# Local attention and two feed-forward layers in fp32: token tiles of 512 and a first one of 256, attention for two blocks at a time in parts of the array

## The chip, the cores and the metric

One core of a Trainium2 chip runs the whole kernel. The metric is the device time of one execution in microseconds (us). A profiled execution gives the rows quoted below; all times in a row are us unless it says ns.

## The reference

Three stages over 2304 tokens (4 sequences of 576) of 512 features (8 heads of 64):

```python
# 1. causal attention with a window of 64 keys
scores = q @ k.T / sqrt(64); mask = (rel >= 0) & (rel < 64)      # rel = query position - key position
x = softmax(where(mask, scores, -1e9)) @ v                       # heads side by side: (2304, 512)
# 2. first feed-forward layer
h = maximum(x @ w_in1, 0); x = (h * h) @ w_out1                  # 512 -> 2048 -> 512
# 3. second feed-forward layer
h = x @ w_in2; out = (h * cos(h)) @ w_out2                       # 512 -> 2048 -> 512
```

Everything is fp32. The feed-forward products are made of three passes each: both operands are split into a high part (rounded by a cast to fp32r) and a low part (the rest), and high*high, high*low and low*high are added in PSUM.

## The kernel before

**Work and tiles.** The tokens are in 6 tiles of 384 (TILE), a tile in 6 attention blocks of 64 queries (QT). The hidden 2048 features are in 16 chunks of 128 (CH). All four split weights of one layer stay in SBUF; the second layer's replace the first's during the last tile of the first. Features are in partitions, tokens in columns.

**Attention of a block** of 64 queries looks at 128 keys (the block's own and the 64 before). `qk` (L333) multiplies, for each of 4 head pairs, a stationary matrix of 128x128 in which the queries of one head fill the upper left quarter and those of the other the lower right, with zeros elsewhere, by 128 key columns. `mask_max` (L669, L674) on DVE scales, masks and takes the row maximum, `exps` (L496) on ACT exponentiates and sums, `invert` and `norm` (L680, L682, L703) on DVE divide, `turn` (L346) on PE transposes, `copy_turned` (L504) on ACT copies to SBUF, `pv` (L361) on PE multiplies the values of both heads (128 keys x 128) by 128 columns of weights, of which the two diagonal 64x64 quarters are used, and `x_high` (L513, ACT) and `x_low` (L689, DVE) split those into x_hi and x_lo, each in two pieces of 64 partitions.

**Feed-forward.** `up` (L371) is 12 matmuls of 384 columns for one chunk; `down1` (L401) is 12 matmuls of 384 columns with the weights stationary; `down2` (L427) is 9 matmuls of 512 columns with the activations stationary, so its output has tokens in partitions. Between them stand, in layer 1, `relu1` (L536, ACT), `square` (L724, DVE), `g_high` (L542, ACT) and `g_low` (L729, DVE); in layer 2 `count_turns` (L563, ACT), three DVE operations (L762, L765, L768), `cosines` (L571, ACT), `times_cos` (L774, DVE), `g_high` and `g_low`.

**What sets the order.** Each engine's program is written out by hand, and semaphores join them. PE does the attention of all 6 blocks of tile 0 first, and only then `up1(0, 0)`. From there a step is `up1(f)`, `down1(f - 2)`, and in tiles 0 to 4 one of `turn` and `qk`, or `pv`, for the next tile's blocks in between. In tile 0 each step also has two weight pieces of 256 KB to take in: SP loads them through three buffers (L248), ACT casts the high part (`w_high`, L529), DVE subtracts (`w_low`, L709). The tiles 1 to 4 of layer 1 and 0 to 4 of layer 2 are hardware loops. Layer 1's result goes to DRAM in fp32 (`store_x2`) and is loaded and split again for layer 2.

```python
for i in range(QT + 4):                       # PE, tile 0
    ...
    if 4 <= i:
        pv(0, i - 4, v0_bank[(i - 4) % 4])
up1(0, 0, 0)
up1(0, 1, 0)
tile1(0, 0, 1)
```

Of the kernel before, what the change touches and what calls it, by code (L numbers as in the profile page):

```python
# [6 lines left out]
def attention_ffn_ffn(nc, q_blocks, k_cols, v_rows, w_in1, w_out1, w_in2, w_out2, x2_dram, out):  # L25
# [5 lines left out]
    P = 128  # L31
    NBLK, _, PAIRS, BLK = q_blocks.shape
    TOKENS, D = v_rows.shape
    WIN = 2 * BLK
    HD = P // 2
    SEQ_BLOCKS = 9
    SCALE = float(HD) ** -0.5
    MASKED = -1000000000.0
    CH = w_in1.shape[0]
    KC = D // P  # L40
    TILE = 384
    TILES = TOKENS // TILE
    QT = TILE // BLK
    TB = TILE // P
    LAG = 2
    L2 = TILES * CH
    SLOTS = 3
    WSLOTS = 3
# [5 lines left out]

    ANGLE_MAX, ANGLE_MIN = HALF_PI - 1e-6, -3 * HALF_PI + 1e-6

    with ExitStack() as ctx:
# [9 lines left out]

        w_in_hi = sb("w_in_hi", [P, KC, CH * P], f32r)
        w_in_lo = sb("w_in_lo", [P, KC, CH * P], f32r)
        w_out_hi = sb("w_out_hi", [P, CH, D], f32r)  # L70
        w_out_lo = sb("w_out_lo", [P, CH, D], f32r)
        w_raw = sb("w_raw", [P, WSLOTS, D])

        x_hi = sb("x_hi", [P, 2, KC, TILE], f32r)
        x_lo = sb("x_lo", [P, 2, KC, TILE], f32r)

        g_hi = sb("g_hi", [P, 2, TILE], f32r)
        g_lo = sb("g_lo", [P, 2, TILE], f32r)

        SLOT = 3 * D  # L80
        work = sb("work", [P, 2 * SLOT])
        relu = work[:, 0:2 * TILE].rearrange("p (s c) -> p s c", s=2)
        act = work[:, 2 * TILE:4 * TILE].rearrange("p (s c) -> p s c", s=2)
        y_stage = work[:, 4 * TILE:8 * TILE]

        arena = sb("arena", [P, SLOTS * (SLOT + PAIRS * WIN) + 2 * PAIRS * P])
        at = [0]

        def carve(n, start=None):
            if start is not None:  # L90
                at[0] = start
            at[0] += n
            return arena[:, at[0] - n:at[0]]

        def qkv(place):

            q, k = (place[:, n * D:(n + 1) * D].rearrange("p (a c) -> p a c", a=PAIRS) for n in range(2))
            return q, k, place[:, 2 * D:3 * D]

        slots = [qkv(carve(SLOT)) for _ in range(SLOTS)] + [qkv(work[:, n * SLOT:(n + 1) * SLOT]) for n in range(2)]  # L100

        slot0 = [0, 1, 2, 3, 4, 0]
        TILE0_USED = [6, 2, 3]
        prob = carve(SLOTS * PAIRS * WIN).rearrange("p (s a c) -> p s a c", s=SLOTS, a=PAIRS)
        prob_t = carve(2 * PAIRS * P).rearrange("p (s a c) -> p s a c", s=2, a=PAIRS)
        x2_raw = carve(KC * TILE, 0).rearrange("p (k c) -> p k c", k=KC)
        turns = carve(2 * TILE).rearrange("p (s c) -> p s c", s=2).bitcast(i32)
        cosine = carve(2 * TILE).rearrange("p (s c) -> p s c", s=2)
# [3 lines left out]
        neg_max = sb("neg_max", [P, SLOTS, PAIRS])  # L112
        row_sum = sb("row_sum", [P, SLOTS, PAIRS])
        inv_sum = sb("inv_sum", [P, SLOTS, PAIRS])
# [5 lines left out]
        y_bank = [ps(f"y{d}") for d in range(KC)]  # L120
        s_bank = ps("scores")
        t_bank = ps("turned")
        h2_bank = h_bank + [s_bank, t_bank]

        s0_bank, t0_bank, v0_bank = (s_bank, y_bank[0]), (t_bank, y_bank[1]), y_bank[2:] + h_bank
# [4 lines left out]
        zeros_set = sem("zeros_set")  # L130
# [14 lines left out]
        pv_done = sem("pv_done")  # L145
        xhi_set = sem("xhi_set")
        xlo_set = sem("xlo_set")
        w_loaded = [sem(f"w_loaded{n}") for n in range(WSLOTS)]
        whi_set = sem("whi_set")
        wlo_set = sem("wlo_set")  # L150
        up_done = sem("up_done")
# [789 lines left out]
```

## Time and profile before

| | |
|---|---|
| Time, median of 3 runs (lowest to highest) | 911.57 us (910.73 to 912.2) |
| The profiled execution: its own time, its span | 912.68 us, 910.9 us |
| PE (matmul) busy | 890.9 us, 98% |
| PEld (weight load) busy | 847.9 us, 93% |
| DVE busy | 524.8 us, 58% |
| ACT busy | 394.2 us, 43% |
| DMA | 54.68 MB, mean 60 GB/s |
| First feed-forward matmul begins | 30.97 us |

A timeline row is: start, duration, engine, source line, operation, output and inputs, partitions x columns, count; in square brackets the idle time before it and what ended it. The duration of a matmul holds the time through the array, in which the next ones already run: what a matmul costs in a dense stretch is the distance from its start to the next start. One fp32 matmul of the program is two instructions in the trace (x8 for four), an fp32r matmul or a transpose is one.

### The profile page before, as it was taken

The page shows a single profiled execution, that of the slowest core. Times are in us where ns is not written, and L with a number is a line of the kernel's source. Part 1 is how long each engine was busy: PE and PEld are TensorE (multiplying, and loading weights), DVE is VectorE, ACT ScalarE, POOL GpSimd, SP SyncE. Part 2 cuts the span into 40 slices and gives each one's busy share as a digit, 9 for nine tenths or more (in the row PEclk, how much of TensorE's full clock was granted, in tenths as well). Part 3 has the DMA queues.
Part 4 walks back from the last instruction along what each step waited for, and adds up shares of the span by engine and source line. Part 5 has one row for each costly group of instructions (what it writes and reads, how often), then busy time and mean ns, then how long its engine had stood idle before and what let it go on. Part 6 is the DMA issues. An engine that isn't in the chain of part 4 may idle for free.

```text
span 910.9 us, 14676 instructions
## 1 busy us (share of the span) xinstructions
PE 890.9 (98%) x5040; PEld 847.9 (93%) x5040; DVE 524.8 (58%) x1028; ACT 394.2 (43%) x967; POOL 2.4 (0%) x13
## 2 busy tenths in 40 slices
PE   6899899999999999999999999999999999999998
PEld 6798899999999999999999999999899999989997
DVE  7666644535444443544375766665665666666664
ACT  6665534434433443344255533433433433433433
POOL 1000000000000000000000000000000000000000
PEclk9999999999999999999999999999999999999999
DMA  6544412221221121120354310010000010000000
GB/s 196 157 121 146 150 59 59 58 59 63 58 60 60 58 58 58 63 58 0 105 158 124 124 35 1 35 35 0 35 35 0 35 35 0 35 0 0 36 1 35
DMA packets 57119, 54.68 MB, mean 60 GB/s; under 512 B 22592, under 2 KB 40512, under 8 KB 57088
## 3 DMA queue, kind: packets, MB, share of 16 engines
q1 hardware_dynamic: 56560, 54.15, 19.1%
q8 instruction: 18, 0.29, 0.1%
q10 hardware_dynamic: 528, 0.13, 0.1%
q14 instruction: 13, 0.11, 0.0%
HBM read 44.83 MB, written 9.44 MB: 60 GB/s over the span
## 4 chain that ended last, share of the span: by engine, by line
PE 90%; DVE 3%; DMA 3%; ACT 2%; issue 1%; SPq 1%
PE h L371 31%; PE y L427 22%; PE y L401 19%; PE turned L371 6%; PE scores L371 6%; PE turned L361 3%; PE scores L333 2%; PE turned L346 1%; DMA w_raw<-w_in 1%; ACT arena L496 1%; DMA w_raw<-w_out 1%; DMA arena<-q_blocks 0%; DVE arena L669 0%; DVE neg_max L674 0%; DVE g_lo L729 0%
## 5 line engine op out<-in xcount | busy, mean ns | idle before, releaser
L371 PE MATMUL h<-x_hi,w_in_hi 128*128 (+1 forms) x576 | 199.2, 346 | 1.7 <-DVE x_lo L689 1.7
L371 PE MATMUL h<-x_hi,w_in_lo 128*128 (+1 forms) x576 | 193.9, 337 | 0.0
L371 PE MATMUL h<-x_lo,w_in_hi 128*128 (+1 forms) x576 | 193.6, 336 | 0.0
L729 DVE TENSOR_TENSOR g_lo<-work,g_hi 128x384 fp32r<-128x384 f32 x192 | 106.4, 554 | 135.2 <-ACT g_hi L542 135.2
L542 ACT CAST g_hi<-work 128x384 fp32r<-128x384 f32 x192 | 97.2, 506 | 104.6 <-PE y L401 84.1
L401 PE MATMUL y<-g_hi,w_out_lo 128*128 128x384 f32 x384 | 128.4, 334 | 0.0
L401 PE MATMUL y<-g_lo,w_out_hi 128*128 128x384 f32 x384 | 128.3, 334 | 0.0
L401 PE MATMUL y<-g_hi,w_out_hi 128*128 128x384 f32 x384 | 128.3, 334 | 0.0
L427 PE MATMUL y<-w_out_hi,g_lo 128*128 128x512 f32 x288 | 113.9, 396 | 0.0
L427 PE MATMUL y<-w_out_lo,g_hi 128*128 128x512 f32 x288 | 113.7, 395 | 0.0
L371 PEld LDWEIGHTS h<-x_hi,w_in_hi 128*128 128x128 f32 x576 | 109.0, 189 | 4.0 <-DVE x_lo L689 1.9
L427 PE MATMUL y<-w_out_hi,g_hi 128*128 128x512 f32 x288 | 111.9, 389 | 0.0
L371 PEld LDWEIGHTS h<-x_lo,w_in_hi 128*128 128x128 f32 x576 | 108.8, 189 | 2.0
L371 PEld LDWEIGHTS h<-x_hi,w_in_lo 128*128 128x128 f32 x576 | 108.5, 188 | 0.0
L571 ACT ACTIVATE arena<-work,half_pi 128x384 f32<-128x384 f32 x96 | 59.3, 617 | 109.0 <-DVE work L768 109.0
L536 ACT ACTIVATE work<-h 128x384 f32<-128x384 f32 x96 | 47.2, 491 | 134.7 <-PE h L371 134.6
L724 DVE TENSOR_TENSOR work<-work 128x384 f32<-128x384 f32 x96 | 53.4, 556 | 65.8 <-ACT work L536 65.6
L401 PEld LDWEIGHTS y<-g_hi,w_out_hi 128*128 128x128 f32 x384 | 72.1, 188 | 0.0
L401 PEld LDWEIGHTS y<-g_hi,w_out_lo 128*128 128x128 f32 x384 | 72.1, 188 | 0.0
L401 PEld LDWEIGHTS y<-g_lo,w_out_hi 128*128 128x128 f32 x384 | 72.1, 188 | 0.0
L427 PEld LDWEIGHTS y<-w_out_hi,g_lo 128*128 128x128 f32 x288 | 54.0, 187 | 11.5
L427 PEld LDWEIGHTS y<-w_out_lo,g_hi 128*128 128x128 f32 x288 | 54.0, 187 | 9.2
(96 smaller groups left out, 1179.7 us busy)
## 6 DMA issues: line engine op xcount, KB each, us to landing
arena<-k_cols SPq DMA_DIRECT2D x33, 256.0 KB, 3.4
arena<-v_rows SPq DMA_DIRECT2D x33, 256.0 KB, 3.4
w_raw<-w_in SPq DMA_DIRECT2D x32, 256.0 KB, 3.6
w_raw<-w_out SPq DMA_DIRECT2D x32, 256.0 KB, 2.7
x_tiles<-work SPq DMA_DIRECT2D x6, 768.0 KB, 3.3
arena<-x_tiles SPq DMA_DIRECT2D x6, 768.0 KB, 4.4
arena<-q_blocks SPq DMA_DIRECT2D x68, 64.0 KB, 2.3
out<-work SPq DMA_DIRECT2D x5, 768.0 KB, 3.5
```

The source lines that it names most:

```text
L333: mm = pe.matmul(bank[:, a * WIN:(a + 1) * WIN], q[:, a, :], k[:, a, :], start=True, stop=True)
L346: mm = pe.transpose(bank[:, a * P:(a + 1) * P], prob[:, i % SLOTS, a, :], ident[:, :])
L361: mm = pe.matmul(bank[:, a * P:(a + 1) * P], v[:, a * P:(a + 1) * P], prob_t[:, i % 2, a, :], start=True, stop=True)
L371: mm = pe.matmul(bank[:, 0:TILE], w[:, k, cols], x_at(x, par, k), start=(n == 0), stop=(n == 3 * KC - 1))
L401: mm = pe.matmul(y_bank[d][:, 0:TILE], w[:, f, cols], g[:, f % 2, :], start=(f == 0 and n == 0), stop=(f == CH - 1 and n == 2))
L427: mm = pe.matmul(y_bank[b][:, 0:D], g[:, f % 2, cols], w[:, f, :], start=(f == 0 and n == 0), stop=(f == CH - 1 and n == 2))
L496: e = nc.scalar.activation(p, p, ACT.Exp, bias=neg_max[:, i % SLOTS, a:a + 1], accum_out=row_sum[:, i % SLOTS, a:a + 1])
L536: nc.scalar.activation(relu[:, f % 2, :], h_bank[f % 2][:, 0:TILE], ACT.Relu).then_inc(relu_set, 1)
L542: nc.scalar.copy(g_hi[:, f % 2, :], act[:, f % 2, :]).then_inc(ghi_set, 1)
L571: nc.scalar.activation(cosine[:, f % 2, :], relu[:, f % 2, :], ACT.Sin, bias=half_pi[:, 0:1]).then_inc(cos_set, 1)
L724: nc.vector.tensor_tensor(act[:, f % 2, :], relu[:, f % 2, :], relu[:, f % 2, :], ALU.mult)\
L729: nc.vector.tensor_tensor(g_lo[:, f % 2, :], act[:, f % 2, :], g_hi[:, f % 2, :].bitcast(fp32), ALU.subtract).then_inc(glo_set, 1)
```

## The change

The tokens are in one tile of 256 and four of 512. In the 256 tile two chunks are handled in one step, side by side in one PSUM bank, so that ACT and DVE work on 512 columns everywhere. Attention is done for two blocks at a time (a duo). `qk` multiplies 64x64 stationary matrices by 128 columns, the one head in the upper left and the other in the lower right quarter of the array, with no zero filling. `pv` multiplies 128x64 stationary matrices by 64 columns, the heads in the two column halves. One `x_high` and one `x_low` on all 128 partitions serve a duo. PE does only duos 0 and 1 (the 256 tile) and `qk(2)` before the first `up1`; duos 2 to 5 come in the 8 steps of the 256 tile, four duos in the 16 steps of each 512 tile after that.

Weights come in pieces of 512 KB through two buffers, 16 for a layer; the first three are split by POOL (`w_split`). A duo's queries and keys are one DMA of 640 KB, its values one of 512 KB. ACT squares (`g_high1`) from the relu result itself, and DVE squares in place for `g_low`. Layer 1's result is split into x_hi and x_lo right from PSUM (`y_high`, `y_low`); its last two tiles stay in SBUF and are the first of layer 2, the others go through DRAM already split. All loops are written out. The range of each engine's program: PE 3901 rows (1964 before), ACT 494 (413), DVE 746 (539), SP 84 (204).

```diff
-    TILE = 384
-    LAG = 2
-    SLOTS = 3
-    WSLOTS = 3
+    WIDE = 512
+    HALF = 256
+    FIRST_DUOS = 2
+    RAW1, RAW2 = 2, 4
+    SIZE = [HALF] + [WIDE] * ((TOKENS - HALF) // WIDE)
+    ORDER = [TILES - 2, TILES - 1] + list(range(1, TILES - 2)) + [0]
...
-                for a in range(PAIRS):
-                    mm = pe.matmul(bank[:, a * WIN:(a + 1) * WIN], q[:, a, :], k[:, a, :], start=True, stop=True)
+                for a in range(PAIRS):
+                    for b in range(2):
+                        for head in range(2):
+                            rows, to = slice(head * HD, (head + 1) * HD), head
+                            mm = pe.matmul(score_bank(2 * d + b)[to * HD:(to + 1) * HD, a * WIN:(a + 1) * WIN],
+                                           q_at[d % 2][rows, a, b * BLK:(b + 1) * BLK],
+                                           k_at[d % 2][rows, a, b * BLK:b * BLK + WIN],
+                                           start=True, stop=True, tile_position=(head * HD, to * HD))
...
-                for a in range(PAIRS):
-                    mm = pe.matmul(bank[:, a * P:(a + 1) * P], v[:, a * P:(a + 1) * P],
-                                   prob_t[:, i % 2, a, :], start=True, stop=True)
+                for b in range(2):
+                    pe.wait_ge(prob_t_set, 2 * d + b + 1)
+                    for a in range(PAIRS):
+                        for head in range(2):
+                            place = head
+                            mm = pe.matmul(pv_bank(d)[head * HD:(head + 1) * HD,
+                                                      (b * PAIRS + a) * BLK:(b * PAIRS + a + 1) * BLK],
+                                           v_at[d % 2][:, b, a * P + head * HD:a * P + (head + 1) * HD],
+                                           prob_t[:, b, a, place * BLK:(place + 1) * BLK],
+                                           start=True, stop=True, tile_position=(0, head * HD))
...
+            for s in range(WSTEPS):
+                up1(s)
+                if s % 2 == 0 and s > 0:
+                    pv(FIRST_DUOS + s // 2 - 1)
+                if s % 2 == 0 and s < WSTEPS - 2:
+                    qk(FIRST_DUOS + s // 2 + 1)
+                if s % 2 == 1:
+                    turn(2 * FIRST_DUOS + s - 1)
+                    turn(2 * FIRST_DUOS + s)
+                if s > 0:
+                    down1(s - 1)
...
+            def w_split(n):
+                _, hi, lo, raw = piece(n)
+                pool.wait_ge(w1_loaded[n % RAW1], 16 * (n // RAW1 + 1))
+                nc.gpsimd.tensor_copy(hi, raw).then_inc(whi_first, 1)
+                pool.wait_ge(whi_first, n + 1)
+                nc.gpsimd.tensor_tensor(lo, raw, hi.bitcast(fp32), ALU.subtract).then_inc(wlo_first, 1)
```

How the instructions stand. PE from its first instruction to the first feed-forward matmul, before (L333 is qk, L346 turn, L361 pv, L371 up):

```order
L333 MATMUL scores<-arena 128x128 x4
L333 MATMUL y<-arena 128x128 x4
L333 MATMUL scores<-arena 128x128 x4
L333 MATMUL y<-work 128x128 x4
...
L346 MATMUL y<-ident,arena 128x128 x4
L361 MATMUL y<-arena,work 128x128 x4
L361 MATMUL y<-arena 128x128 x4
L371 MATMUL h<-x_hi,w_in_hi 128x384
```

and the same place in the change (L341 is qk, L355 turn, L365 pv, L385 up):

```order
L341 MATMUL y<-arena 64x128 x32
L355 MATMUL scores<-ident,arena 128x128 x4
L355 MATMUL turned<-ident,arena 128x128 x4
L365 MATMUL y<-arena 64x64 x16
L355 MATMUL scores<-ident,act 128x128 x4
L355 MATMUL turned<-ident,act 128x128 x4
L365 MATMUL y<-arena 64x64 x16
L341 MATMUL y<-arena 64x128 x16
L385 MATMUL h<-x_hi,w_in_hi 128x256
```

Four blocks instead of six stand ahead of the first `up`, and the scores of two more; the qk of one duo is 16 matmuls of 128 columns where two blocks had 8, its pv 16 of 64 columns where two blocks had 8 of 128.

PE in the second tile of layer 1, change: the qk of duo 6 stands between the 12 matmuls of `up` and the 12 of the next chunk's, all of 512 columns now:

```order
L385 MATMUL h<-x_hi,w_in_lo 128x512
L341 MATMUL scores<-arena 64x128 x2
L341 MATMUL turned<-arena 64x128 x2
L341 MATMUL scores<-arena 64x128 x2
L341 MATMUL turned<-arena 64x128 x2
...
L385 MATMUL h<-x_hi,w_in_hi 128x512
```

There each of `qk` and `pv` is entered from and left to full-array matmuls once for a duo.

DVE in an odd step of the change's first tile (L708 is square, L715 g_low, L672 and L677 mask_max, L703 w_low, L682 to L687 norm):

```order
L708 TENSOR_TENSOR act<-act 128x512
L715 TENSOR_TENSOR g_lo<-act,g_hi 128x512
L672 SCALAR_TENSOR_TENSOR arena<-y,masks 128x512
L677 TENSOR_REDUCE neg_max<-arena 128x4
L703 TENSOR_TENSOR w_in_lo<-arena,w_in_hi 128x1024
L703 TENSOR_TENSOR w_out_lo<-arena,w_out_hi 128x1024
L682 TENSOR_SCALAR row_sum<-row_sum 128x4
L684 RECIPROCAL inv_sum<-row_sum 128x4
L687 TENSOR_TENSOR arena<-arena,inv_sum 128x512
```

Before, a block's softmax and two pieces of 512 columns stood in a pair of steps with two squares and two g_lows; now a block's softmax and two pieces of 1024 columns stand in every step.

## Rows read from the trace of the kernel before

**Rows 1.** The page, busy us, share of the span, instructions.

```profile
PE 890.9 (98%) x5040; PEld 847.9 (93%) x5040; DVE 524.8 (58%) x1028; ACT 394.2 (43%) x967; POOL 2.4 (0%) x13
```

**Rows 2.** Windows, PE alone: length, busy (matmuls), granted clock, DMA share, GB/s.

```profile
4.60:13.60 9.00, 8.14 (x33) 1.00 0.85 218
31.00:110.00 79.00, 73.41 (x449) 0.98 0.52 156
110.00:200.00 90.00, 90.00 (x566) 1.00 0.20 61
600.00:700.00 100.00, 100.00 (x503) 1.00 0.07 24
```

**Rows 3.** Waits of PE: total us, times, longest.

```profile
PE scores L333 <- DMA arena<-q_blocks: 4.8, 2, 4.6
PE turned L346 <- DVE x_lo L689: 4.6, 3, 1.7
```

**Rows 4.** Timeline of PE, layer 1 with attention in between.

```profile
123.33 1.05 PE L333 MATMUL scores<-arena 128*128 128x128 f32 x8
124.14 0.42 PE L371 MATMUL h<-x_hi,w_in_hi 128*128 x1
124.39 0.34 PE L371 MATMUL h<-x_lo,w_in_hi 128*128 x1
...
132.55 0.60 PE L346 MATMUL turned<-ident,arena 128*128 128x128 f32 x4
132.98 1.06 PE L333 MATMUL scores<-arena 128*128 128x128 f32 x8
...
138.04 1.05 PE L361 MATMUL turned<-arena 128*128 128x128 f32 x8
138.85 0.42 PE L371 MATMUL h<-x_hi,w_in_hi 128*128 x1
139.11 0.34 PE L371 MATMUL h<-x_lo,w_in_hi 128*128 x1
```

**Rows 5.** Timeline of PE, dense stretches of layer 1 and at layer 2's end.

```profile
126.48 0.33 PE L401 MATMUL y<-g_lo,w_out_hi 128*128 128x384 f32 x1
...
128.56 0.33 PE L371 MATMUL h<-x_lo,w_in_hi 128*128 x1
...
902.26 0.39 PE L427 MATMUL y<-w_out_lo,g_hi 128*128 128x512 f32 x1
...
907.25 0.39 PE L427 MATMUL y<-w_out_hi,g_lo 128*128 128x512 f32 x1
```

**Rows 6.** Timeline of PE, the start, and the first `up`.

```profile
4.58 2.04 PE L333 MATMUL scores<-arena 128*128 128x128 f32 x8 [4.58 <-DMA arena<-q_blocks]
...
30.97 0.69 PE L371 MATMUL h<-x_hi,w_in_hi 128*128 128x384 f32 x1 [1.73 <-DVE x_lo L689]
...
33.38 0.52 PE L371 MATMUL h<-x_lo,w_in_hi 128*128 128x384 f32 x1
33.70 0.48 PE L371 MATMUL h<-x_hi,w_in_lo 128*128 128x384 f32 x1
```

**Rows 7.** Timeline of weight loads after a qk.

```profile
124.11 0.19 PEld L371 LDWEIGHTS h<-x_hi,w_in_hi 128*128 128x128 f32 x1
124.22 0.19 PEld L371 LDWEIGHTS h<-x_lo,w_in_hi 128*128 128x128 f32 x1
```

**Rows 8.** The page, DMA issues: count, KB each, us to landing.

```profile
w_raw<-w_out SPq DMA_DIRECT2D x32, 256.0 KB, 2.7
...
arena<-x_tiles SPq DMA_DIRECT2D x6, 768.0 KB, 4.4
```

**Rows 9.** Timeline of DVE and ACT, tile 0.

```profile
39.25 0.69 DVE L669 SCALAR_TENSOR_TENSOR arena<-scores,masks 128x512 f32<-128x512 f32 x1
40.58 0.55 DVE L724 TENSOR_TENSOR work<-work 128x384 f32<-128x384 f32 x1
...
43.55 0.62 ACT L529 CAST w_out_hi<-w_raw 128x512 fp32r<-128x512 f32 x1
```

More of the change, by code:

```diff
@@ L95, in qkv @@
[L95 to L105, printed above, removed]
@@ new lines, in _ @@
+            qk(0)
+            qk(1)
+            pe.wait_ge(ident_set, 1)
+            turn(0)
+            turn(1)
+            pv(0)
+            turn(2)
+            turn(3)
+            pv(1)
+            qk(2)
+            for s in range(WSTEPS):
+                up1(s)
[8 more added lines that the diff above has]
+                    down1(s - 1)
@@ L869, in _ @@
[L869 to L880 removed]
+            mask_max(0)
@@ new lines, in _ @@
+            mask_max(1)
+            norm(0)
+            mask_max(2)
+            norm(1)
+            mask_max(3)
+            norm(2)
+            x_low(0)
+            norm(3)
+            x_low(1)
+            mask_max(4)
+            mask_max(5)
+            norm(4)
+            for s in range(WSTEPS):
+                d = FIRST_DUOS + s // 2
+                if s == 0:
+                    norm(5)
+                square(s)
+                g_low(s)
+                if s % 2 == 0 and s > 0:
+                    x_low(d - 1)
+                if d + 1 < EARLY_DUOS:
+                    t = 2 * (d + 1) + s % 2
+                    mask_max(t)
+                for n in pieces1_of(s):
+                    w_low(n)
+                if d + 1 < EARLY_DUOS:
+                    norm(2 * (d + 1) + s % 2)
@@ new lines, in _ @@
+            x_low(EARLY_DUOS - 1)
+            for g in range(first1[1], G1):
+                j, s, _ = steps1[g]
+                d = START[min(j + 1, TILES - 1)] // (2 * BLK) + s // 4
+                if j + 1 < TILES:
+                    if s % 4 == 0:
+                        mask_max(2 * d)
+                    if s % 4 == 1:
+                        norm(2 * d)
+                square(g)
+                g_low(g)
+                if s == 0:
+                    y_low(j - 1)
+                if j + 1 < TILES:
+                    if s % 4 == 0:
+                        mask_max(2 * d + 1)
+                    if s % 4 == 1:
+                        norm(2 * d + 1)
+                    if s % 4 == 3:
+                        x_low(d)
+                else:
+                    for n in pieces2_of(s):
+                        w_low(n)
@@ new lines, in _ @@
+            for g in range(G2):
+                i, s, _ = steps2[g]
+                if g > 0:
+                    g_low(G1 + g - 1)
+                angles(g)
+                if g == 0:
+                    y_low(TILES - 1)
+                if g < 2:
+                    for n in pieces2_of(2 * WSTEPS + g):
+                        w_low(n)
+                if s == 1 and i > 0:
+                    y2_copy(i - 1, 1)
+                    y2_copy(i - 1, 3)
+                times_cos(g)
+            g_low(G1 + G2 - 1)
```

1138 lines of the change are left out of this document (522 added, 616 removed).

## The prediction

> **What bounds the kernel now.** The page says it first: PE is busy 890.9 of 910.9 us [rows 1]. The windows say where it isn't: from 110 us on every window is full, between 31 and 110 us (most of tile 0) 5.6 us are lost, and before 31 us PE only does attention [rows 2]. The waits of PE name the gaps: the first loads, then turn waiting for DVE's x_lo [rows 3]. So the end is set by the sum of PE's own work, plus the start until the first `up`. DVE and ACT matter in the start and in tile 0 alone. I therefore price everything by the distance between matmul starts, not by the durations in the rows.
>
> Those distances. In layer 1 twelve matmuls of 384 columns take from 126.48 to 128.56, 0.1733 each; at the end 22 of 512 columns take from 902.26 to 907.25, 0.2268 each [rows 5]. 384 columns at 2.4 GHz are 0.160, 512 are 0.2133: in both cases 0.0133 is left over. So a matmul costs its columns and 13.3 ns, and wider matmuls save the 13.3 ns. A step of layer 2 (21 matmuls) takes 100 x 21 / 503 = 4.175 [rows 2], against 12 x 0.1733 + 9 x 0.2268 = 4.12, so 0.05 of disturbance, which I leave as it is. In layer 1 a step is 24 x 0.1733 = 4.16.
>
> Attention of a block: `qk` begins at 123.33, the second matmul after it at 124.39; less one 0.173 it costs 0.89. `pv` the same way (138.04, 139.11) 0.90. `turn` to the next `qk` (132.55, 132.98) 0.43 [rows 4]. Together 2.21 a block.
>
> The sum closes: 30.97 to the first `up` [rows 6], 30 blocks x 2.21 = 66.3, 96 steps x 4.16 + 96 x 4.175 = 800.2, the first nine matmuls at 0.32 instead of 0.173 (1.3) [rows 6], 5.6 idle [rows 2], is 904.4; the last matmul ends at 907.64 [rows 5], so 3.2 stays unexplained, and 3.3 goes from there to the end of the span. I carry both over.
>
> **The start.** The zero filling by DVE and the many small loads go away, but the first qk needs 640 KB where the old one had three small loads, and the second duo's 640 KB come in beside it. A load of 256 KB takes 2.7, of 768 KB 4.4 [rows 8], so 512 KB more cost 1.7; 1280 KB should take about 6.1 after an issue at 0.7, and qk(0) starts at about 6.7 instead of 4.58. PE is slow there: four matmuls (eight instructions) take 2.04 [rows 6] instead of 0.89, and the first `up` matmuls are 0.32 apart [rows 6], which is 384 columns at 1.2 GHz: the lower clock level by its spacing, though the granted clock of that window reads 1.00 [rows 2]. Four blocks' scores end near 13.7, as before. From there it is a chain through DVE and ACT, of 1.33 for a mask and maximum (39.25 to 40.58 [rows 9]), some 1.6 for four exponentials, 1.0 for a norm. Laid out in the written order, norm(3) ends near 21.7, pv(1) near 24.3, its x_low near 25.7. qk(2) waits for that and costs 1.8: first `up` at 27.5. Before it was 30.97, with six blocks done instead of four.
>
> **Attention after the start**, in 16 duos. Turns: 8 transposes each, 0.86, 13.8 in all. qk: 16 matmuls of 128 columns in a duo. If the two quarters run side by side that is the time of 8, 1.77; 15 of them 26.6. If they don't, twice that. pv: 16 matmuls of 64 columns. With halves side by side and everything in step with the columns 0.89; if weight loads or the halves come one after the other, 1.79, the same as two old pv. Rows show two weight loads of 128 columns 0.11 apart [rows 7], so 64 columns could be loaded in 0.055, four of them to a pair of matmuls: that alone would give 1.76 if the two halves' loads can't overlap. I take 1.3, between the ends: 20.8 in all (14.2 to 28.6).
>
> Entering and leaving these modes is 4 changes a duo, 64 in all. The trace has no such change. Its nearest rows are the change from fp32 to fp32r, after which the first matmul is 0.25 instead of 0.173 from the next, so 0.08 (124.14 to 124.39 [rows 4]), and an emptied array: a matmul of 384 columns lasts 0.33, 0.16 more than its distance [rows 5]. With the weight load of 0.19 [rows 7] not hidden either it would be 0.35. Nothing below: a change can't save time. I take 0.12, between the two nearest: 7.7 (0 to 22). The Trainium skill (TensorEngine Tiling (Array Packing), section Key Properties) says that changing the tiling mode drains TensorE. With a full 0.16 a change the sum would be 2.5 higher. No run yet shows the drain.
>
> **Feed-forward.** The columns stay the same. The matmuls become fewer: 5 x 16 x 12 instead of 6 x 16 x 12 for each layer's `up` and for `down1`, 576 less in all, at 13.3 ns: 7.7 saved, 800.2 becomes 792.5. This needs 256 columns to take 0.120. An fp32 instruction of qk has its own weight load and takes 0.111 (0.89/8 [rows 4]), so the load alone allows it; the other end is that the loads need the 0.173 they have now, which would cost the 576 matmuls of 256 columns 31. I take 0.120. The cold matmuls after the start stay, 1.3.
>
> **First tile, 8 steps.** PE has per step 48 x 0.120 = 5.76 and some 2.2 of attention, 8.0. DVE and ACT now pass a block through in each step: square and g_low 1.35, mask 1.33, exponentials 1.7, w_high 0.95, w_low twice 1.1 each, norm 1.0, and x_low in every second step; these follow one another across both engines (exponentials wait for the mask, w_low for w_high, the norm stands behind both w_low) and add up to about 9.0. The 1024-column costs are estimates, from 512 columns at 0.69 and 384 at 0.55, 0.62 for the cast [rows 9]. For six steps PE loses 1.0 each, with hops 7 in all, where 5.6 were lost before.
>
> **Later tiles.** ACT and DVE have 5.5 a step and need about 3.3 at most; y_high and y_low at a tile's end have the 2.7 of an `up` and a `down`. Nothing. At the very end the chain from the last `up` through cos to g_low is some 0.1 longer per operation, and the change no longer issues the last two `up` together: 0.5.
>
> **The sum:** 27.5 + 13.8 + 26.6 + 20.8 + 7.7 + 792.5 + 1.3 + 7 + 0.5 + 3.2 + 3.3 = 904.2 of span, against 910.9. The profiled execution's own time was 1.8 over its span and 1.1 over the median of the runs, so 904.9 us.
>
> **The rivals.** *A, all overlaps, changes free:* pv at 0.89 and no cost of a change, 904.9 - 6.6 - 7.7 = 890.6. For it: the trace shows weight loads hidden everywhere. Against: such short matmuls stand nowhere in it. 18%.
>
> *B, changes dear:* 0.35 each and pv at 1.79: 904.9 + 14.7 + 7.8 = 927.4, slower. For it: the 13.3 ns that are left at every weight change say that a handover costs something even without a change of mode. Against: attention's fp32 stretches are entered for 0.08. 12%.
>
> *C, the two quarters of qk don't run side by side,* and this is the one on the other side that I can name a place for: qk 3.55 a duo. It costs 26.6 after the start, and in the start, on the path, twice 3.55 (at the lower level) and 1.8: 940.4. Its point: from half an overlap on (13 + 4) the change loses. In this kernel both quarters write the same bank at the same time, in different partitions, which the old qk never did. The Trainium skill (TensorEngine Tiling, Gotcha 1: PSUM Pressure) says that different row tiles can't access one PSUM bank simultaneously, and by that rule it would be this case; the same skill (TensorE: Matmul & The Clock Gate, Part 3) gives 10.6 times for 16 tiles, with (section Why this matters for your kernels) a bank for each row of tiles. Nothing in the trace decides it. 12%.
>
> *D, tile 0 starved:* two buffers of 512 KB; a piece is loaded (3.6, from the loads of 256 and 768 KB [rows 8]) between w_low in one step and w_high in the next, some 7 apart. SP's queue is written in order, and POOL's splits of the first three pieces, for which the trace has no price, stand ahead of pieces 3 and 4. If each of six steps lacks 2 more: 904.9 + 12 = 916.9. For it: waits of this sort exist [rows 3]. Against: 218 GB/s were reached [rows 2], about 170 are needed. 8%.
>
> The forecast keeps 50%.
>
> **How the numbers follow.** A measurement of this kernel can tell about 0.2% from no change, 1.8 us: faster means below 909.7. The forecast's own range is 897 to 912 (pv and changes towards their ends, 2 to 12 lost in tile 0), of which some 8 parts in 10 are faster. With A that gives 0.61 faster; some of D's mass and the forecast's upper edge give 0.07 the same; B, C, most of D and the rest 0.32 slower. The range for 8 in 10 takes A and B in and leaves C out: 889 to 928.
>
> **What would show it.** In the profile after: the first `up` at 27 to 28; distances of 0.120 and 0.2268 in the feed-forward stretches; a qk of a duo at 1.8 from start to next `up`, a pv at 0.9 to 1.8; PE idle of 3 to 10 in the first tile and nearly none behind it. Wrong it would be if qk takes 3.5 (C), if the matmul next to a change starts more than 0.2 late (B), if 256 columns take over 0.13, or if the windows of the first 100 us show more than 15 idle (D).

## The result and the profile after

The change makes the kernel slower by 0.4%: 915.67 us, the median of 8 runs (913.68 to 918.51), beside 911.74 (910.48 to 913.07, 8 runs) of the kernel before. The ratio is 1.0044, with a 95% interval of 1.0029 to 1.006. The profiled execution took 915.88 us, its span is 913.7 us. The forecast was 904.9 and faster: the time lies in its range of 889 to 928, the direction is wrong.

The page first, the line that answers to [rows 1]:

```profile
PE 877.4 (96%) x5040; PEld 736.4 (81%) x5040; DVE 474.4 (52%) x761; ACT 363.1 (40%) x762; POOL 12.7 (1%) x19
```

PE is busy 13.5 less than before, and yet the span is 2.8 longer. So the work did become cheaper, and more than that went into waiting: PE is idle for 36.3 of its span, where it was for 20.0. The windows say where. PE alone, columns as in [rows 2], first of the kernel after:

```profile
0.00:30.00 30.00, 12.59 (x144) 0.84 0.58 211
30.00:60.00 30.00, 25.03 (x246) 0.87 0.35 114
60.00:90.00 30.00, 23.17 (x220) 0.94 0.37 124
90.00:120.00 30.00, 26.80 (x256) 0.94 0.43 150
118.00:510.80 392.80, 392.25 (x2365) 1.00 0.20 66
510.80:910.50 399.70, 399.51 (x1850) 1.00 0.07 24
```

and the same of the kernel before:

```profile
30.00:60.00 30.00, 27.88 (x166) 0.94 0.57 175
60.00:90.00 30.00, 28.14 (x179) 1.00 0.43 126
90.00:120.00 30.00, 27.42 (x168) 1.00 0.45 134
```

From 118 us on PE is full, as forecast. From 30 to 120 it is idle for 15.0 where it was idle for 6.6, its granted clock is 0.87 to 0.94, and the DMA engines move *less* than before (114 and 124 GB/s in the first two windows, 175 and 126 before). Something upstream of both is late. The waits of PE in the whole span, against [rows 3]:

```profile
PE y L341 <- DMA arena<-qk_duos: 13.6, 3, 6.2
PE h L385 <- DVE w_in_lo L703: 6.5, 3, 2.2
PE scores L355 <- DVE arena L687: 4.4, 1, 4.4
PE turned L355 <- DVE arena L687: 3.6, 1, 3.6
...
PE scores L355 <- DVE x_lo L697: 1.0, 1, 1.0
```

One of the three waits for queries and keys is the start (6.2). The other two (7.4) and the three for w_in_lo (6.5) are in the first tile, and [rows 3] had neither there.

**Two marks in PE's timeline** cut the sum into pieces, the first `up` and the first `up` of tile 1:

```profile
30.07 3.68 PE L341 MATMUL y<-arena 64*64 64x128 f32 x32 [1.50 <-DVE x_lo L697]
33.68 0.58 PE L385 MATMUL h<-x_hi,w_in_hi 128*128 128x256 f32 x1
...
115.12 0.40 PE L385 MATMUL h<-x_hi,w_in_hi 128*128 128x512 f32 x1
```

By the forecast's terms they stand at 27.5 and 97.5 (27.5, 8 steps x 5.76, 1.3 and 7, and 15.6 of attention: 3 qk, 4 pv, 4 duos' turns and their 14 mode changes). Measured they are at 33.68 and 115.12. So the start lost 6.2 and the first tile 11.4. From the second mark to the end of the span the terms give 806.7, and it took 798.6: 8.1 better than forecast. 904.2 + 6.2 + 11.4 - 8.1 = 913.7.

**The start.** POOL splits the first pieces (CAST, then TENSOR_TENSOR); here are its rows

```profile
9.93 2.35 POOL L829 TENSOR_TENSOR w_in_lo<-arena,w_in_hi 128x1024 fp32r<-128x1024 f32 x1
...
13.34 2.34 POOL L829 TENSOR_TENSOR w_in_lo<-arena,w_in_hi 128x1024 fp32r<-128x1024 f32 x1
...
17.21 2.35 POOL L829 TENSOR_TENSOR w_out_lo<-arena,w_out_hi 128x1024 fp32r<-128x1024 f32 x1
```

and those of DVE beside them:

```profile
10.04 0.69 DVE L672 SCALAR_TENSOR_TENSOR arena<-y,masks 128x512 f32<-128x512 f32 x1 [9.12 <-PE y L341]
...
13.44 0.18 DVE L684 RECIPROCAL inv_sum<-row_sum 128x4 f32<-128x4 f32 x1
13.65 2.58 DVE L687 TENSOR_TENSOR arena<-arena,inv_sum 128x512 f32<-128x512 f32 x1
...
17.47 2.11 DVE L682 TENSOR_SCALAR row_sum<-row_sum 128x4 f32<-128x4 f32 x1
```

The norm (L687) took 2.58 where it takes 0.69 elsewhere, and a TENSOR_SCALAR of 4 columns 2.11 where it takes 0.17. Both begin while a subtraction of POOL runs. The small one ends with it (19.58 and 19.56), the norm 0.55 after it (16.23 and 15.68), as if it had begun only then. The mask (10.04), in the middle of the first subtraction, keeps its 0.69, and so does the reciprocal (13.44, inside the second) its 0.18. Together the norm and the small operation lost 3.8 in DVE's queue; how much of that reached the first `up` runs 1 and 10 show. The other large piece is `qk(2)`, at 30.07: 3.6 instead of 1.8, at the lower clock level (granted clock 0.50 from 30.1 to 33.6).

**The first tile.** One step of it. PE's rows first:

```profile
64.56 0.60 PE L355 MATMUL turned<-ident,arena 128*128 128x128 f32 x4
...
70.19 0.39 PE L385 MATMUL h<-x_hi,w_in_hi 128*128 128x256 f32 x1 [2.16 <-DVE w_in_lo L703]
...
79.07 3.41 PE L341 MATMUL y<-arena 64*64 64x128 f32 x32 [4.67 <-DMA arena<-qk_duos]
```

then DVE's

```profile
64.84 0.69 DVE L672 SCALAR_TENSOR_TENSOR arena<-y,masks 128x512 f32<-128x512 f32 x1 [4.21 <-PE scores L355]
...
68.91 1.23 DVE L703 TENSOR_TENSOR w_in_lo<-arena,w_in_hi 128x1024 fp32r<-128x1024 f32 x1 [2.66 <-ACT w_in_hi L544]
```

ACT's

```profile
66.29 0.40 ACT L512 ACTIVATE arena<-arena,neg_max 128x128 f32<-128x128 f32 x1 [8.42 <-DVE neg_max L677]
...
67.85 1.03 ACT L544 CAST w_in_hi<-arena 128x1024 fp32r<-128x1024 f32 x1
```

and SP's queue:

```profile
70.16 0.33 SPq L252 DMA_DIRECT2D arena<-w_in  x1
...
71.67 1.21 SPq L243 DMA_DIRECT2D arena<-v_duos  x1
72.92 0.43 SPq L238 DMA_DIRECT2D arena<-qk_duos  x1
```

Read in order of time this is a circle. The next duo's mask (64.84) waits for this duo's `turn`, because `prob` (the tile that holds the masked scores and then the weights of the softmax) has room for one duo: DVE stands idle for 4.21 before it and ACT for 8.42. `w_high` is written behind the exponentials, and waits there, though its piece lies in SBUF. `w_low` (68.91) waits for `w_high`, and PE's next `up` for `w_low` (2.16). Only `w_low`'s end frees the piece's buffer, so SP issues the next piece's load then (70.16, 71.30), and the loads of v and of the next queries and keys, which wait for nothing of that, stand behind it in the queue: they go out at 71.67 and 72.92, and `qk` waits 4.67 for them. That qk makes the next turn late, and the turn the next mask. From one turn to the one two steps on (64.56 to 88.71) it takes 24.2, where the forecast's terms give some 18. Behind some of the waits PE runs at the lower clock level: the `qk` at 79.07 takes 3.41 instead of 1.96, and after the wait of 2.16 before 47.93 fifteen matmuls of 256 columns start 0.213 apart, which is 256 columns at 1.2 GHz (granted clock 0.50 from 48.0 to 51.3). Not behind all of them: after the wait of 2.16 before 70.19 they start 0.12 apart at once (granted clock 1.00 from 70.2 to 73.0). What decides between the two, these rows don't show.

**The steady tiles** went by the terms. PE around a pv and a qk, layer 1:

```profile
213.45 0.39 PE L385 MATMUL h<-x_hi,w_in_lo 128*128 128x512 f32 x1
213.77 1.15 PE L365 MATMUL scores<-arena 128*64 128x64 f32 x32
214.85 0.50 PE L413 MATMUL y<-g_hi,w_out_hi 128*128 128x512 f32 x1
215.19 0.39 PE L413 MATMUL y<-g_lo,w_out_hi 128*128 128x512 f32 x1
...
220.52 0.44 PE L341 MATMUL scores<-arena 64*64 64x128 f32 x4
...
222.41 0.50 PE L413 MATMUL y<-g_hi,w_out_hi 128*128 128x512 f32 x1
222.75 0.40 PE L413 MATMUL y<-g_lo,w_out_hi 128*128 128x512 f32 x1
```

A qk is 1.89, a pv 1.08. The distance into a mode is 0.32 and out of it 0.34, where 0.227 is the matmul's own, so a change costs 0.09 to 0.11 (the matmul's own 0.227 taken off). With the turns (233.24 to 234.57 less two matmuls, 0.88) a duo costs 1.89 + 1.08 + 4 x 0.10 + 0.88 = 4.25, where [rows 4] give 4.42 for two blocks. The new modes save under 0.2 a duo, some 3 us in all.

### The profile page after: what moved, and what is told of

The parts are those of the page before. It is cut to its first block, busy times and chain, and to the rows that moved or that the text cites. A ratio compares the mean times of both kernels' runs of the same rounds, so it can differ in the third digit from the quotient of the medians.

```text
span 913.7 us, 12478 instructions
## 1 busy us (share of the span) xinstructions
PE 877.4 (96%) x5040; PEld 736.4 (81%) x5040; DVE 474.4 (52%) x761; ACT 363.1 (40%) x762; POOL 12.7 (1%) x19
## 4 chain that ended last, share of the span: by engine, by line
PE 90%; DVE 5%; DMA 2%; ACT 2%; issue 0%; SPq 0%; DVEq 0%; ACTq 0%
PE h L385 31%; PE y L452 21%; PE y L413 21%; PE turned L385 5%; PE scores L385 5%; DMA arena<-qk_duos 2%; PE y L341 2%; PE scores L365 2%; PE scores L341 1%; PE turned L341 1%; PE turned L355 1%; ACT arena L512 1%; PE scores L355 1%; DVE w_in_lo L703 1%; DVE neg_max L677 1%; DVE arena L687 1%
## 5 line engine op out<-in xcount | busy, mean ns | idle before, releaser
L385 PE MATMUL h<-x_hi,w_in_hi 128*128 128x512 f32 (+1 forms) x480 | 178.8, 372 | 6.5 <-DVE w_in_lo L703 6.5
L385 PE MATMUL h<-x_lo,w_in_hi 128*128 128x512 f32 (+1 forms) x480 | 177.9, 371 | 0.0
L385 PE MATMUL h<-x_hi,w_in_lo 128*128 128x512 f32 (+1 forms) x480 | 177.9, 371 | 0.0
L708 DVE TENSOR_TENSOR act<-act 128x512 f32<-128x512 f32 x72 | 49.6, 690 | 156.3 <-ACT g_hi L556 156.3
L715 DVE TENSOR_TENSOR g_lo<-act,g_hi 128x512 fp32r<-128x512 f32 x144 | 99.7, 692 | 51.9 <-ACT g_hi L561 49.5
L413 PE MATMUL y<-g_hi,w_out_hi 128*128 128x512 f32 (+1 forms) x320 | 122.3, 382 | 0.5 <-DVE x_lo L722 0.5
L413 PE MATMUL y<-g_lo,w_out_hi 128*128 128x512 f32 (+1 forms) x320 | 118.2, 369 | 0.0
L413 PE MATMUL y<-g_hi,w_out_lo 128*128 128x512 f32 (+1 forms) x320 | 117.9, 368 | 0.0
L385 PEld LDWEIGHTS h<-x_hi,w_in_hi 128*128 128x128 f32 x480 | 91.9, 191 | 23.1 <-DVE w_in_lo L703 7.1
L385 PEld LDWEIGHTS h<-x_hi,w_in_lo 128*128 128x128 f32 x480 | 91.9, 191 | 15.0
L385 PEld LDWEIGHTS h<-x_lo,w_in_hi 128*128 128x128 f32 x480 | 91.8, 191 | 14.9
L589 ACT ACTIVATE arena<-arena,half_pi 128x512 f32<-128x512 f32 x72 | 52.2, 725 | 129.3 <-DVE arena L742 129.3
L512 ACT ACTIVATE arena<-arena,neg_max 128x128 f32<-128x128 f32 x136 | 52.8, 390 | 68.2 <-DVE neg_max L677 68.2
L452 PEld LDWEIGHTS y<-w_out_hi,g_hi 128*128 128x128 f32 x288 | 54.1, 188 | 12.0 <-DVE g_lo L715 1.0
```

Source lines behind the costliest of these rows:

```text
L385: mm = pe.matmul(bank[:, c * size:(c + 1) * size], w[:, f // 2, k, cols], x_of(x, j, parity)[:, k, :], start=(n == 0), stop=(n == 3 * KC - 1))
L413: mm = pe.matmul(bank, w[:, f // 2, f % 2, d * P:(d + 1) * P], x[:, g % 2, c * size:(c + 1) * size], start=(s == 0 and c == 0 and n == 0 a ...
L452: mm = pe.matmul(y_bank[b][:, :], x[:, g % 2, cols], w[:, f // 2, f % 2, :], start=(s == 0 and c == 0 and n == 0), stop=(last and c == len ...
L512: e = nc.scalar.activation(of[:, a, :], of[:, a, :], ACT.Exp, bias=neg_max[:, t % 4, a:a + 1], accum_out=row_sum[:, t % 4, a:a + 1])
L589: nc.scalar.activation(cosine[:, g % 2, :], angle[:, g % 2, :], ACT.Sin, bias=half_pi[:, 0:1]).then_inc(cos_set, 1)
L708: nc.vector.tensor_tensor(a, a, a, ALU.mult).then_inc(sq_set, 1)
```

## The experiments

Three places to mend are taken one by one (1 to 3) and together (4, 5); two try the order of the weights and the cold clock (6, 7); the last three measure prices that the forecast had to guess (8 to 10), from one execution each. Times are medians; the last column is the span less the second mark, and the marks are those of the profiled execution. The kernel before was timed again beside each group of runs: its median was 911.74 beside the change, 912.96 beside runs 1, 2, 3 and 5, 911.71 beside 4, 7, 8 and 9, and 911.88 beside 6 and 10. So runs of two groups are better compared by their ratios.

| Run | us (runs) | ratio to the kernel before, 95% | first `up` | tile 1's first `up` | rest |
|---|---|---|---|---|---|
| the change | 915.67 (8) | 1.0044 (1.0029 to 1.006) | 33.68 | 115.12 | 798.6 |
| 1 e1_no_pool | 915.48 (12) | 1.0025 (1.0014 to 1.0036) | 31.13 | 111.95 | 799.7 |
| 2 e2_loads_first | 908.18 (5) | 0.9953 (0.994 to 0.9966) | 34.00 | 107.17 | 798.5 |
| 3 e3_weights_first | 903.34 (6) | 0.9896 (0.9878 to 0.9915) | 34.72 | 105.52 | 798.6 |
| 4 e4_loads_weights | 901.96 (5) | 0.9892 (0.9875 to 0.991) | 34.28 | 102.11 | 798.6 |
| 5 e5_all_three | 900.31 (4) | 0.9856 (0.9839 to 0.9874) | 30.65 | 100.02 | 799.7 |
| 6 e10_between | 903.67 (6) | 0.9915 (0.9896 to 0.9934) | 31.09 | 102.21 | 799.7 |
| 7 e6_qk2_late | 905.73 (6) | 0.9929 (0.9911 to 0.9948) | 27.38 | 105.23 | 799.1 |
| 8 e7_qk_by_head | 946.88 (1) | | 35.31 | 129.75 | 815.0 |
| 9 e8_pv_by_head | 921.54 (1) | | 33.54 | 116.06 | 803.3 |
| 10 e9_pool_writes_only | 913.82 (1) | | 29.39 | 113.01 | 798.7 |

The last column is the first finding: in every version that leaves the steady tiles alone, what follows tile 1's first `up` takes 798.5 to 799.7 (the 0.5 to 1.1 more in the four with run 1's edit was not followed up). All that the runs 1 to 7 gain or lose lies before it.

**1. POOL's splits given to ACT and DVE** (`e1_no_pool`):

```diff
+                nc.scalar.copy(hi, raw).then_inc(whi_first, 1)
...
+                nc.vector.tensor_tensor(lo, raw, hi.bitcast(fp32), ALU.subtract).then_inc(wlo_first, 1)
...
-            for n in range(EARLY):
-                w_split(n)
```

> The splits of the first three weight pieces are taken from POOL: ACT casts, DVE subtracts, between their start-up operations. Theory P (while POOL's subtraction of 2.35 us reads SBUF, DVE operations that need the second read path stand still; this holds up the start): norm(0) takes 0.69 instead of 2.58 and the small operation of norm(1) 0.16 instead of 2.11, the first up begins 3 us earlier or so (30 to 31.5 instead of 33.7), the time falls by 2 to 4 us against the changed kernel, to about 912 to 913. Rival (the start is set by the loads and the ACT chain, DVE's stalls are hidden): first up stays within 1 us of 33.7 and the three splits of 1.2 us that DVE now has make it later.

The norm took 0.69 again and the small operation 0.16. The first `up` came 2.6 earlier and tile 1's 3.2; the circle was untouched (12.8 for queries and keys with the start's 6.3, 7.9 for w_in_lo). The time of 912 to 913 was missed (915.48). Its ratio is 0.2% under the change's, and the intervals just overlap: by the trace the blocked DVE is real, but it is the smaller part, and alone it leaves the change slower than before.

**2. Attention's loads ahead of the weights in SP's queue** (`e2_loads_first`):

```diff
-                for n in pieces1_of(s + 1):
-                    load_piece(n)
...
+                if s in (1, 3, 5):
+                    load_qk(5 + s // 2)
+                if s in (2, 4, 6):
+                    load_v(3 + s // 2)
+                for n in pieces1_of(s + 1):
+                    load_piece(n)
```

> In the first tile SP issues the loads of queries, keys and values ahead of the weight pieces of the same step. Theory Q (qk waits because its load stands in SP's queue behind weight pieces that wait for w_low): PE's waits for qk_duos in the first tile fall from 7.4 to under 1 us, the time by 3 to 8 us, to 908 to 913. Rival (the tile is bound by DMA bandwidth or by the DVE and ACT chain): the same time is lost elsewhere, as a longer wait for w_in_lo, and the total moves by less than 1 us.

The longest wait of PE from 34 to 119 us:

```profile
PE h L380 <- DVE w_in_lo L698: 7.9, 4, 2.2
```

No qk of the first tile waits for its load any more; the waits for w_in_lo stayed (7.9 in four, 6.5 in three before the edit). This edit alone turns the loss into a gain of 0.5%.

**3. The weights ahead of the next duo's softmax** (`e3_weights_first`), on ACT and DVE:

```diff
-                if d + 1 < EARLY_DUOS:
-                    exps(2 * (d + 1) + s % 2)
                 for n in pieces1_of(s):
                     w_high(n)
+                if d + 1 < EARLY_DUOS:
+                    exps(2 * (d + 1) + s % 2)
```

(on DVE `w_low` goes ahead of `mask_max` the same way).

> In the first tile's steps ACT and DVE split the weights before the mask, maximum and exponentials instead of behind them. Theory W (w_low stands behind mask_max, which waits for turn, which stands behind up on PE: a circle through three engines): the waits of up for w_in_lo, 6.5 us, go, and since SP's loads are freed earlier the waits for qk_duos shrink as well; time down 4 to 10 us, to 906 to 912. Rival (DVE's and ACT's sum of work sets the tile): softmax comes out late instead, turn waits for norm by about as much, total within 2 us of the changed kernel.

The two longest there:

```profile
PE y L341 <- DVE arena L672: 4.6, 2, 2.5
PE scores L355 <- DVE x_lo L697: 1.8, 1, 1.8
```

Both waits of the circle are gone, that for w_in_lo *and* that for the queries and keys, although SP's order was left as it was. With the pieces done early their buffers come free early, and the queue is not held up. What is new is a wait of qk for the mask (its bank must have been read), which now stands behind both subtractions. It is the strongest single edit: 1% faster than the kernel before, and 12.3 us under the change, where 4 to 10 were expected.

**4. Both** (`e4_loads_weights`):

> Loads first and weights first together, POOL's splits kept. The runs with one of them each gave 908.2 and 903.3 us where the change has 915.7. If both remove the same circle (SP's load behind w_low, w_low behind the mask), together they give little more than weights first alone: 901 to 904. If they are separate losses they add: about 896. Against the run with all three (900.3) this tells what POOL's splits cost once the first tile no longer waits: 2 to 3 us by the 2.6 us that the first up came earlier without them.

Tile 1's first `up` comes 3.4 earlier than in run 3. Alone, the edits brought it forward by 8.0 and 9.6 us, together by 13.0 and not 17.6: they cut the same circle in two places, and the second cut is worth less. The profiled execution of run 3 is its slowest; by the medians it is 7.5 and 12.3 alone and 13.7 together, which says the same more strongly. In the medians run 4 can't be told from run 3 (0.9892 and 0.9896), whose runs are further apart (900.3 to 906.24). Their times go with the mean granted clock: 906.0 and 906.24 us at 0.984, 902.74 to 903.92 at 0.990, 900.3 at 0.994. To run 5, which also takes POOL's splits away, it lacks 1.7 us in the medians, or 0.4% in the ratios (2 to 3 us expected).

**5. All three** (`e5_all_three`):

> The three edits together: no POOL splits, loads first, weights first. If the losses of the first 115 us are these three queues (theories P, Q, W), the second tile's first up comes 12 to 20 us earlier than at 115.1, the time is 896 to 904 and both before and the change are beaten. If instead the array modes or the 256-column matmuls cost the time, it stays above 910.

The windows of PE:

```profile
30.00:60.00 30.00, 26.97 (x281) 0.99 0.54 175
60.00:90.00 30.00, 27.86 (x281) 0.94 0.52 175
```

and what it waits for most between the first `up` and tile 1:

```profile
PE y L336 <- DVE arena L675: 5.2, 2, 3.0
```

In the second and third windows PE is idle for 5.2, where it was for 11.8. Over the whole first tile it is idle for 7.0: qk waits 5.2 for the mask, in two waits, and a turn 1.8 for x_lo. The DMA engines are back at 175 GB/s. Tile 1 begins 15.1 earlier (12 to 20 expected), and the median is 15.4 lower. From the first `up` to tile 1's it takes 69.4, where the forecast's terms give 70.0. At 900.31 us this beats both kernels, the one before by 1.4%.

**6. The softmax between the two pieces** (`e10_between`), on top of run 5, to take away its wait for the mask: ACT and DVE do one piece, then the exponentials or the mask, then the other piece.

```diff
-                for n in pieces1_of(s):
+                for n in pieces1_of(s)[:1]:
...
+                for n in pieces1_of(s)[1:]:
+                    w_high(n)
```

> All three edits, with the mask, maximum and exponentials between the two weight pieces of a step instead of behind both. In the version with all three (900.3 us) qk still waits 5.2 us in the first tile for the mask of the duo before and turn 1.8 for x_low. If the two splits ahead of the mask (1.2 us each on DVE, 0.95 on ACT) are why, those waits fall by 2 to 4 and the time to 897 to 899. If the order inside a step no longer matters because a step's sum on DVE and ACT is what's left, it stays at 900 within 1.

Both expectations missed: it is 3.4 slower than run 5 (by the ratios 0.6%, and the intervals don't overlap). The waits from 34 to 119 us:

```profile
PE y L336 <- DVE arena L677: 4.7, 2, 2.4
PE scores L350 <- DVE x_lo L702: 3.4, 1, 3.4
```

The wait for the mask hardly shrank (4.7), and the second piece's `w_high` now stands behind the exponentials once more, so the operations after it are later: the last `turn` of the tile waits 3.4 instead of 1.8 for x_lo. The mask isn't late for the subtraction ahead of it alone; which step sets it was not followed up.

**7. qk(2) after the first `up`** (`e6_qk2_late`), on top of run 5:

```diff
-            qk(2)
             for s in range(WSTEPS):
                 up1(s)
+                if s == 0:
+                    qk(2)
+                if s == 1:
+                    qk(3)
...
-                if s % 2 == 0 and s < WSTEPS - 2:
+                if s % 2 == 0 and 0 < s < WSTEPS - 2:
```

> All three edits, and qk of duo 2 behind the first up instead of ahead of it (qk of duo 3 one step later too). Theory S: qk(2) stands in the start on the path, 3.6 us at the lower clock level; taken off, the first up begins at 27 to 27.5 instead of 30.65, and the time falls by 1 to 3 us to 897 to 899, since some of it comes back as a later mask for duos 2 and 3. Rival: duo 2's softmax, now later by an up at the lower level, is what the first tile waits for next; no change or up to 2 us slower than 900.3.

The first `up` comes 3.3 earlier than in run 5, at 27.38, and tile 1's 5.2 later; the time is 5.4 us longer (0.7% by the ratios). Theory S missed, and the rival had the direction but at most 2 us. PE at the first `up`:

```profile
27.38 0.58 PE L380 MATMUL h<-x_hi,w_in_hi 128*128 128x256 f32 x1 [1.41 <-DVE x_lo L703]
27.75 0.41 PE L380 MATMUL h<-x_lo,w_in_hi 128*128 128x256 f32 x1
...
32.57 1.96 PE L336 MATMUL y<-arena 64*64 64x128 f32 x32
```

Now nearly the whole first `up` runs 0.213 apart, at 1.2 GHz (granted clock 0.50 from 27.4 to 32.0); in run 5 `qk(2)` stood there at 0.50 (27.1 to 30.6), and the first `up` behind it ran 0.12 apart from its second matmul on. So in these two executions the cold stretch was moved, not removed, and the scores of duo 2 came later (32.57 instead of 27.04). That this lateness is what costs the 5.2 at tile 1 fits, but was not tried by itself.

**8. qk, all of one quarter, then all of the other** (`e7_qk_by_head`):

```diff
-                for a in range(PAIRS):
-                    for b in range(2):
-                        for head in range(2):
+                for head in range(2):
+                    for a in range(PAIRS):
+                        for b in range(2):
```

> The changed kernel with the 16 matmuls of a qk in another order: all 8 of the upper left quarter first, then all 8 of the lower right one, instead of in turn. If the 1.75 us of a qk (8 times 0.22) come from two quarters that work at the same time, they can't overlap now and a qk takes about 3.5 us; 12 of them in the dense tiles cost 21 us, all 18 some 30, time 940 to 950. If matmuls of a quarter are simply cheaper than full ones and don't overlap, nothing changes.

PE around one qk:

```profile
213.13 0.43 PE L341 MATMUL scores<-arena 64*64 64x128 f32 x2
213.40 0.38 PE L341 MATMUL turned<-arena 64*64 64x128 f32 x2
...
216.39 0.51 PE L413 MATMUL y<-g_hi,w_out_hi 128*128 128x512 f32 x1
```

From start to the next mode 3.26 instead of 1.89, with the same matmuls. So alternating quarters do overlap, though both write one bank, in different partitions. Whether two matmuls run at a time, or one matmul and the other quarter's weight load, the run doesn't tell: an instruction takes 0.109 in a row and 0.055 alternating, and its 128 columns at 2.4 GHz are 0.053. The marks say where the 31.2 more went: 16.4 behind tile 1's first `up`, which is 12 qk x 1.37; 13.0 in the first tile, where two of its three qk ran at the lower clock level (6.17 and 6.29); and only 1.6 in the start. The Trainium skill (TensorEngine Tiling (Array Packing), Gotcha 1: PSUM Pressure) says that different row tiles can't access the same PSUM bank simultaneously. Taken as a ban on any overlap that doesn't hold here, by 1.89 against 3.26; if only the weight loads overlap, the sentence stands.

**9. pv by head** (`e8_pv_by_head`): the same exchange of loops in pv.

```diff
-                    for a in range(PAIRS):
-                        for head in range(2):
+                    for head in range(2):
+                        for a in range(PAIRS):
```

> The same for pv: for each block the 4 matmuls of one column half, then the 4 of the other. If the 1.08 us of a pv (34 ns an instruction) come from halves that overlap, a pv takes 1.8 to 2.2 us now (32 instructions of 55 to 67 ns), 13 to 20 us more in all. If 34 ns is what issuing an instruction costs, it stays at 1.1.

A pv took 1.47 (215.90 to 217.37) instead of 1.08, between the two expectations. 12 x 0.39 is 4.7, and the last column is 4.7 longer; 5.9 more were measured in all. Its 32 instructions are 46 ns each in a row and 34 ns alternating: the column halves overlap (matmuls or weight loads, as in run 8), but save a quarter, where the diagonal quarters of qk save 42%.

**10. POOL only writes** (`e9_pool_writes_only`). The low parts of layer 1's first three pieces are left out: POOL writes zeros in their place.

```diff
-                nc.gpsimd.tensor_tensor(lo, raw, hi.bitcast(fp32), ALU.subtract).then_inc(wlo_first, 1)
+                nc.gpsimd.memset(lo.bitcast(fp32), 0.0).then_inc(wlo_first, 1)
```

> The changed kernel with POOL's subtraction for the first three weight pieces replaced by writing zeros into the same low part, so POOL no longer reads two SBUF operands there (their low part is left out, as far as the first layer's two chunks pairs use it). If POOL's reading is what stops DVE (theory P, narrower), norm(0) takes 0.69 and the small operation of norm(1) 0.16 even where they fall into a POOL instruction, and the first up begins near 31, as without POOL's splits (31.1). If any long POOL instruction stops DVE, a DVE operation inside the zero writing stays as long as it lasts, 1 to 2 us.

POOL and DVE in the timeline, and `qk(2)` on PE:

```profile
15.78 1.04 POOL L827 CAST w_out_hi<-arena 128x1024 fp32r<-128x1024 f32 x1 [2.23 <-DMA arena<-w_out]
...
16.18 1.20 DVE L687 TENSOR_TENSOR arena<-arena,inv_sum 128x512 f32<-128x512 f32 x1
...
16.88 0.95 POOL L829 MEMSET w_out_lo<- 128x1024 f32 x1
...
27.50 1.96 PE L341 MATMUL y<-arena 64*64 64x128 f32 x32 [1.50 <-DVE x_lo L697]
```

The one norm that met a CAST of POOL (which reads SBUF) took 1.20, 0.51 longer, where the cast still ran for 0.64. No norm began under a MEMSET, so whether POOL's writes hold one up stays open; this one ended 0.5 after a MEMSET had begun beside it, and not later than the cast explains. The first `up` was 4.3 earlier, but not all of that is POOL's subtractions: `qk(2)` began 2.6 earlier (27.50 for 30.07), and it ran at the upper clock level here (granted clock 1.00, 1.89 to the first `up` for 3.6), behind the same wait of 1.50. In run 1, where it ran at the lower level, it also began 2.6 earlier (27.52). So the subtractions cost the start 2.6, and the level at which `qk(2)` runs 1.7. The Trainium skill (SBUF — State Buffer, section Who interferes with whom) says that a DVE instruction with two SBUF inputs contends with a GpSimd instruction that reads SBUF, and that the second to issue is fully blocked for the other's length, while one with at most one SBUF input isn't, unless it runs in one of DVE's modes with two ports, which a TENSOR_SCALAR can enter. The rows agree: 2.58 and 1.20 for the norm, which reads `arena` and `inv_sum`, 0.69 for the mask, which reads one bank of PSUM and `masks`, 0.18 for the reciprocal, which reads only `row_sum`. The TENSOR_SCALAR reads only `row_sum` too, beside a constant, and took 2.11; the mode it ran in no row shows. By that rule the stalls of the norm could have been forecast from the change's own order of POOL and DVE.

## Why the prediction was wrong, step by step

- **What bounds the kernel, and pricing by distances:** right. 0.120 a matmul of 256 columns (35.24 to 35.36 and on), 0.2267 of 512 (620.22 to 625.66 for 24).
- **qk, pv, turns and mode changes:** right within their sizes. qk 1.89 a duo for 1.77 (+1.8 in 15), pv 1.08 for 1.3 (-3.5 in 16), a change about 0.10 for 0.12 (-1.3 in 64). Rivals A, B and C fall: overlap is real but not free, changes cost a third of B's price, and a qk takes 1.89 and not C's 3.55 (run 8 shows the overlap). The full drain of 0.16, which was weighed for a change, is more than the 0.10 measured.
- **"The start", 27.5:** failed, measured 33.68. The loads were right (first qk at 6.24, forecast 6.7), and the four blocks' scores ended at 12.0 instead of 13.7. But pv(1)'s x_low ended at 29.9 instead of 25.7. The chain assumed DVE's durations undisturbed; POOL's splits were counted as no work on the path, and cost 2.6 of these 4.2 (runs 1 and 10; by the rows DVE stood still for 3.8). The other 1.6 of the chain no run takes apart. And `qk(2)` was priced at 1.8, at full clock: it took 3.6. In run 10 it took 1.89 at the same place, so this price depends on the clock level it meets. The working of this term also reads a granted clock of 1.00 for the window of the first `up` before; that 1.00 is the window from 4.60 to 13.60, and from 31.00 to 33.70 it is 0.50, as the spacing of 0.32 says.
- **"First tile, 8 steps", 7 lost:** failed, and this is the larger error. The forecast added DVE's and ACT's operations up to a step of 9.0 and stopped there. It left out that `mask_max` waits for PE's `turn` with the weights' operations queued behind it, and that SP's queue puts attention's loads behind a piece that waits for `w_low`. The circle through all four engines takes 12 a step. Idle was 14.9 (7.4 + 6.5 + 1.0) instead of 7; the other 3.5 of the 11.4 are mostly matmuls at the lower clock (by their distances 4.7, where the forecast had 1.3). With the circle cut, run 5's first tile takes 69.4 and idles for 7.0, the forecast's 70.0 and 7; but its waits are for the mask and x_lo, so that 9.0 is what a step costs is not shown.
- **Rival D, tile 0 starved,** came true in kind: it named the two buffers, SP's order and POOL, and its 12 over the forecast for the first tile is near the 11.4 measured. That its 916.9 is so near to 915.67 is chance, since the start's 6.2 and the 8.1 behind nearly cancel. It had only 8%, and it expected loads to take long; in the trace the DMA engines had time to spare, and the loads were *issued* late. Its sign, 15 idle in the first 100 us, was badly set: the kernel before has 14 in the first 90 already (10.2 before 30 us), the change 29.
- **After the first tile,** 8.1 better than forecast. Of these 5.3 are layer 2's disturbance, which I carried over: before, nine matmuls of 512 columns in layer 2 took 2.08 (620.88 to 622.96), 0.231 each; after, 0.2267. Three quarters of the attention's -3.0 make 2.2; 0.6 is within the 3.2 that stayed unexplained. Why layer 2 is now undisturbed was not tried.
- **The end:** 0.25 lost before the last `down` (907.03 to 907.51), 0.5 forecast.

From tile 1 on the kernel takes 8.1 less than the forecast's terms, so the savings are there. What made it slower is the order in which its start and its first tile were written, and runs 2 to 5 get it back with not one operation less.

## What to carry to other kernels

Where four queues are written by hand, don't add the operations of each engine up: walk once around, and at each wait ask what is queued behind it that doesn't need it. Here loads that waited for nothing stood behind loads that waited for a buffer, and ready weights stood behind a softmax that waited for PE. A block of work that is off the critical path can still hold up the one engine that is on it, so look whether POOL reads SBUF while DVE reads two operands from it, or runs a TENSOR_SCALAR. And what stands right behind a long wait may run at the lower clock; when something else was put there (run 7), the cost moved and did not go away.

## What the runs showed of the hardware

- Two diagonal 64x64 quarters that write one PSUM bank in different partitions overlap, in their matmuls or their weight loads: 16 fp32 matmuls of 128 columns take 1.89 us alternating and 3.26 us in two blocks of one quarter each.
- Column halves with 64 columns a matmul overlap less: 1.08 us alternating, 1.47 us not.
- Going into or out of such a mode costs 0.09 to 0.11 us.
- A DVE instruction of 4 columns can last 2.11 us when it meets a subtraction of POOL (a TENSOR_SCALAR with one tensor as input); a RECIPROCAL of 4 columns inside another one kept its 0.18 us.
- After a wait of 2.16 us the matmuls of 256 columns started 0.213 us apart for 3 us at a granted clock of 0.50, then 0.120 again; after another wait of 2.16 us they started 0.12 us apart at once. `qk(2)` behind a wait of 1.50 us took 3.6 us in the change and in runs 1 and 5, and 1.89 us in run 10.
